# Key-value products of an item ahead of its second scores, with the copies, roundings and rests around the first layer pair and the gates put in another order

## The reference

```python
# 1: retention, B=2 batches, H=8 heads, S=768 steps, D=64
state = gamma * state + einsum('bhd,bhe->bhde', k[:, :, t], v[:, :, t])
y[:, :, t] = scale * einsum('bhd,bhde->bhe', q[:, :, t], state)
# 2: token mixing of rank 32 (U, V), then a two-layer MLP 512 -> 2048 -> 512
u = x + (x^T @ U @ V)^T
x2 = u + max(u @ w_ch1, 0) @ w_ch2
# 3: spatial gating
h = max(x2 @ w_in, 0); u3, v3 = h split in halves
v_s = w_spatial @ layernorm(v3) + b_spatial
out = (u3 * v_s) @ w_out
```

## Time and profile before

| | |
|---|---|
| median of 3 runs | 475.24 us (474.47 to 475.42) |
| the profiled execution | 473.94 us, its span 471.9 us |
| TensorE matmuls | busy 462.0 us, 98% of the span |
| VectorE | busy 339.2 us, 72% |
| ScalarE | busy 251.4 us, 53% |
| GpSimd | busy 48.2 us, 10% |
| the chain that ended last | 91% TensorE, 5% VectorE, 2% ScalarE, 2% transfers |

### The profile page before, as it was taken

One profiled execution on the slowest core, in us unless ns is written; L12 is line 12 of the kernel. 1 busy time (PEld: TensorE's weight loads), 2 busy tenths in 40 slices (PEclk: granted clock), 3 DMA queues, 4 the chain that ended last, 5 costly groups with the idle time before them and its releaser, 6 DMA issues.

```text
span 471.9 us, 8650 instructions
## 1 busy us (share of the span) xinstructions
PE 462.0 (98%) x3140; PEld 411.5 (87%) x3140; DVE 339.2 (72%) x755; ACT 251.4 (53%) x589; POOL 48.2 (10%) x52
## 2 busy tenths in 40 slices
PE   8899998999999999999999999999999999999997
PEld 5788897988999999988888999988888689999997
DVE  4788978887789987874855976774813997794430
ACT  1666755555667655833464655733432855454312
POOL 2178970000000000000100000000100001000000
PEclk9999999999999999999999999999999999999999
DMA  8989801344432343202220343202105002011003
GB/s 282 405 289 315 303 2 45 112 158 133 135 123 91 100 139 121 91 11 78 90 90 1 107 138 115 91 7 84 44 1 200 1 0 92 0 66 69 0 1 135
DMA packets 20361, 50.31 MB, mean 107 GB/s; under 512 B 1504, under 2 KB 3168, under 8 KB 19168
## 3 DMA queue, kind: packets, MB, share of 16 engines
q1 hardware_dynamic: 19904, 49.24, 30.4%
q10 hardware_dynamic: 416, 0.53, 0.3%
HBM read 46.61 MB, written 3.15 MB: 105 GB/s over the span
## 4 chain that ended last, share of the span: by engine, by line
PE 91%; DVE 5%; ACT 2%; DMA 2%; issue 1%; DVEq 0%; ACTq 0%
PE bank L1413 9%; PE bank L1411 9%; PE bank L1414 9%; PE bank L1394 8%; PE bank L1392 8%; PE bank L1395 8%; PE bank L1532 5%; PE bank L1261 3%; PE bank L1513 3%; PE bank L1516 3%; PE bank L1515 3%; PE bank L1451 2%; PE bank L1453 2%; PE bank L1452 2%; PE bank L1306 2%; PE bank L1300 2%
## 5 line engine op out<-in xcount | busy, mean ns | idle before, releaser
L1392 PE MATMUL bank<-bh,w1c 128*128 128x256 f32 x336 | 94.6, 282 | 1.9 <-DVE hl L985 1.9
L1395 PE MATMUL bank<-bh,w1c 128*128 128x256 f32 x336 | 94.7, 282 | 0.0
L1394 PE MATMUL bank<-bl,w1c 128*128 128x256 f32 x336 | 94.6, 282 | 0.0
L1413 PE MATMUL bank<-hl,w2h 128*128 128x512 f32 x192 | 75.9, 395 | 0.0
L1411 PE MATMUL bank<-hh,w2h 128*128 128x512 f32 x192 | 75.8, 395 | 0.0
L1414 PE MATMUL bank<-hh,w2l 128*128 128x512 f32 x192 | 74.7, 389 | 0.0
L1392 PEld LDWEIGHTS bank<-bh,w1c 128*128 128x128 f32 x336 | 63.5, 189 | 8.7 <-issue 2.1
L977 DVE TENSOR_TENSOR c<-bank,p 128x256 f32<-128x256 f32 x72 | 30.5, 424 | 52.6 <-PE bank L1395 31.4
L1394 PEld LDWEIGHTS bank<-bl,w1c 128*128 128x128 f32 x336 | 63.4, 189 | 5.5
L1395 PEld LDWEIGHTS bank<-bh,w1c 128*128 128x128 f32 x336 | 63.4, 189 | 0.0
L614 ACT ACTIVATE p<-bank 128x256 f32<-128x256 f32 x72 | 27.5, 381 | 48.2 <-PE bank L1395 47.1
(11 more groups left out here) (142 smaller groups left out, 933.2 us busy)
## 6 DMA issues: line engine op xcount, KB each, us to landing
w1raw<-w SPq DMA_DIRECT2D x24, 512.0 KB, 5.0
w2raw<-w SPq DMA_DIRECT2D x24, 512.0 KB, 4.1
att<-attn SPq DMA_DIRECT2D x7, 1152.0 KB, 7.8
att<-attn SPq DMA_DIRECT2D x10, 384.0 KB, 5.4
out_T<-stage SPq DMA_DIRECT2D x7, 384.0 KB, 2.4
wsp_raw<-w_sp SPq DMA_DIRECT2D x1, 2304.0 KB, 8.3
winraw<-w_in SPq DMA_DIRECT2D x4, 512.0 KB, 5.0
tab<-decay SPq DMA_DIRECT2D x7, 258.0 KB, 4.8
```

The source lines that it names most:

```text
L1392: mm(o, w1c[k][:, 0, q, s], bh[:, q, c, :], start=(opens and c == 0), stop=False, skip_group_check=True)
L1394: mm(o, w1c[k][:, 0, q, s], bl[:, q, c, :], start=False, stop=False, skip_group_check=True)
L1395: m = mm(o, w1c[k][:, 1, q, s], bh[:, q, c, :], start=False, stop=(c == 1), skip_group_check=True)
L1413: mm(ch_ps[c][:, :], w2h[h][:, s], hl[k][:, h, :], start=False, stop=False, skip_group_check=True)
```

## The change

Only orders and wait counts change; every engine does the same operations on the same tiles. (1) Items 2 to 7: kv(i) goes ahead of scores(i, 1) on TensorE, and states(i) ahead of mask_a(i, 1) on VectorE. (2) First pair: the third piece of the hidden tile (s=2, the one that sits in PSUM) is rounded and rested second, and product(1, 1) waits for two rests instead of three (HID_FIRST gives the new counts); rests of weights 4 to 6 of pair 1, p_rest(7) and u_add(7) go behind sum_c(1, 0) or later; up(7) moves from behind product(1, 0) to behind product(1, 4), and ch2(0, 0) from behind product(1, 1) to behind product(1, 2). (3) relu_in of the last stretch's tiles 0 and 1 goes ahead of round_wsp(0) and round_wsp(1). (4) For gates a = 0 and 2, sp_copy(a+1, 0) goes ahead of round_g(a, 3).

```diff
--- before.py
+++ after.py
@@ -283,6 +283,7 @@
             return kv_ps[:, c * P:(c + 1) * P] if c < NC - 2 else y_ps[1][:, GW:GW + P]
 
 
+        HID_FIRST = (1, 3, 2)
         WIN_AT = ((0, 4), (0, 5), (0, 6), (1, 3))
         PAIRS = NI // B
         NN = NT * NP
@@ -694,7 +695,9 @@
                     copy_pr(n, 0)
                     if n == 0:
                         xn_copy(NI - 1, 1)
-                    elif n > 1:
+                    elif n == 1:
+                        round_w1(n, range(4, NQ))
+                    else:
                         round_w2(n - 1, 1)
                     if n:
                         round_w1(n + 1, range(0, 2))
@@ -703,8 +706,9 @@
                     copy_pr(n, 1)
                     if n == 0:
                         copy_pr(n, 2)
+                    round_w1(n + 1, range(2, 4))
+                    if n == 0:
                         p_round(NI - 1)
-                    round_w1(n + 1, range(2, 4))
                     if final:
                         round_b(t + 1, range(1, 3))
                     if n:
@@ -721,12 +725,12 @@
                         round_b(t + 1, range(4, 5))
                     if t and j == 4:
                         round_x2(t - 1, range(2, 4))
+                    if n == 0:
+                        relu_hid(n, 2)
                     relu_hid(n, 1)
                     if n:
                         round_w2(n, 0)
-                    relu_hid(n, 2)
-                    if n == 0:
-                        round_w1(n + 1, range(4, 7))
+                        relu_hid(n, 2)
                     if final:
                         round_b(t + 1, range(5, 7))
                     if t and j >= 4:
@@ -808,9 +812,9 @@
             round_x2(NT - 1, range(1, CT))
             round_v(0, range(4, NQ))
             set_bias(0, 0)
+            relu_in(NT - 1, range(0, 2))
             round_wsp(0)
             round_wsp(1)
-            relu_in(NT - 1, range(0, 2))
             round_wsp(2)
             relu_in(NT - 1, range(2, 3))
             round_wsp(3)
@@ -824,7 +828,8 @@
             relu_in(NT - 1, range(6, 8))
 
             for a in range(NA):
-                sp_copy(a, 0)
+                if a % 2 == 0:
+                    sp_copy(a, 0)
                 if a:
                     set_bias(a, 1)
                 if a < NA - 1:
@@ -844,6 +849,8 @@
                 round_g(a, 2)
                 if a == 0:
                     round_wout(range(2, CT))
+                if a % 2 == 0:
+                    sp_copy(a + 1, 0)
                 round_g(a, 3)
                 if a == 1:
                     round_v(2, range(NQ))
@@ -978,7 +985,7 @@
 
             def rest_hid(n, s):
                 k = n % 2
-                dve.wait_ge(hid_hi, 3 * n + s + 1)
+                dve.wait_ge(hid_hi, 3 * n + s + 1 if n else HID_FIRST[s])
                 o, x, hi = ((hl[k][:, 1, HT:TW], c22[:, :], raw(hh[k])[:, 1, HT:TW]),
                             (hl[k][:, 0, :], c1[:, :], raw(hh[k])[:, 0, :]),
                             (hl[k][:, 1, 0:HT], pr_ps[k][:, 0:HT], raw(hh[k])[:, 1, 0:HT]))[s]
@@ -1043,9 +1050,12 @@
                                             ALU.subtract).then_inc(ust_lo, 1)
                 xn_rest(i - 1, 0)
                 xn_rest(i - 1, 1)
-                mask_a(i, 1)
+                if i == 1:
+                    mask_a(i, 1)
                 states(i, 0, NC - 2)
                 states(i, NC - 2, NC - 1)
+                if i > 1:
+                    mask_a(i, 1)
                 p_rest(i - 1)
                 if i == 1:
                     dve.wait_ge(vraw_loaded, 16)
@@ -1064,6 +1074,9 @@
                     if t and j == 1:
                         add_x2(t - 1, range(CT))
                     sum_c(n, 0)
+                    if n == 1:
+                        rest_w1(n, range(4, NQ))
+                        p_rest(NI - 1)
                     if t and j == 0:
                         rest_b(t, range(5, NQ))
                     if n == 0:
@@ -1075,7 +1088,7 @@
                     if n == 0:
                         sum_c(n, 1)
                         sum_c(n, 2)
-                        p_rest(NI - 1)
+                        rest_hid(n, 0)
                     weight_sums(n + 1, range(3, 4))
                     if final:
                         rest_b(t + 1, range(0, 1))
@@ -1088,17 +1101,17 @@
                         rest_w1(n + 1, range(4, 5))
                         sum_c(n, 2)
                         rest_w1(n + 1, range(5, 6))
-                    rest_hid(n, 0)
                     if n:
+                        rest_hid(n, 0)
                         rest_w1(n + 1, range(6, 7))
-                    else:
-                        rest_w1(n + 1, range(2, 4))
-                    rest_hid(n, 1)
-                    if n:
+                        rest_hid(n, 1)
                         rest_w2(n, 0)
                     rest_hid(n, 2)
                     if n == 0:
-                        rest_w1(n + 1, range(4, 7))
+                        rest_w1(n + 1, range(2, 3))
+                        rest_hid(n, 1)
+                        rest_w1(n + 1, range(3, 4))
+                    if n == 1:
                         u_add(NI - 1)
                     if final:
                         rest_b(t + 1, range(2, 5))
@@ -1352,9 +1365,12 @@
                 scores(i, 0)
                 turn(i - 1, 0)
                 turn(i - 1, 1)
-                scores(i, 1)
+                if i == 1:
+                    scores(i, 1)
                 kv(i, 0, NC - 2)
                 kv(i, NC - 2, NC - 1)
+                if i > 1:
+                    scores(i, 1)
                 down(i - 1)
                 outputs(i, 0)
                 outputs(i, 1)
@@ -1375,7 +1391,7 @@
                 if n and q == 0:
                     pe.wait_ge(c_sum, 3 * n)
                 if n and q == 1:
-                    pe.wait_ge(hid_lo, 3 * n)
+                    pe.wait_ge(hid_lo, 3 * n if n > 1 else 2)
                 if q == 2:
                     pe.wait_ge(pr_copied, 3 * n + 1)
                 if q == 3:
@@ -1399,7 +1415,7 @@
                 h, c = g // CT, g % CT
                 k, j = n % 2, n % NP
                 if c == 0:
-                    pe.wait_ge(hid_lo, 3 * n + 2 + h)
+                    pe.wait_ge(hid_lo, 3 * n + 2 + h if n else 3)
                     if n == 0:
                         pe.wait_ge(w2_first_lo, h + 1)
                     else:
@@ -1470,10 +1486,14 @@
                         continue
                     product(n, 0)
                     if n == 1:
-                        up(NI - 1)
-                    for q in range(1, 7):
+                        product(n, 1)
+                    for q in range(2 if n == 1 else 1, 7):
                         product(n, q)
-                        ch2(n - 1, q - 1)
+                        if n == 1 and q == 4:
+                            up(NI - 1)
+                        ch2(n - 1, q - (2 if n == 1 else 1))
+                    if n == 1:
+                        ch2(n - 1, 5)
                     ch2(n - 1, 6)
                     ch2(n - 1, 7)
                     if t and j == 4:
```

## The result

| | median | lowest to highest | executions |
|---|---|---|---|
| before | 475.33 us | 474.47 to 475.61 | 4 |
| after | 468.61 us | 468.33 to 469.25 | 4 |

The ratio is 0.9863, 95% interval [0.9846, 0.9881]: 6.7 us faster. The forecast was 471.4 us with a range of 470.2 to 472.9, so the change is faster, as forecast, but by more than the range allowed. The profiled execution took 468.76 us (span 466.7), against 473.94 (span 471.9) before: 5.2 us. That is less than the 6.7 between the medians, and both are more than the 3.85 of the sum.

What follows compares the result with a forecast made beforehand. TensorE's matmuls, filling 462.0 of 471.9 us, were taken as the bound. Terms 0.60 + 1.4 + 0.95 + 0.9 = 3.85 us off the profiled 473.94 gave 470.1; 1.30 added for the median made 471.4, range 470.2 to 472.9.

Steps and rivals of the forecast that it cites:

- 1 items: Items 3 and 7: kv ahead of the second scores covers TensorE's gaps of 0.41 and 0.19; 0.60 us, from 0 to 0.8.
- 2 first pair: Between pairs 0 and 1: product(1, 1) starts 1.91 us earlier, less 0.52 for moved up(7); 1.4 us, from 1.1 to 1.86.
- 3 input product: Last stretch's input product: TensorE's 0.92 us wait for a relu behind two roundings closes; 0.95 us, from 0.6 to 1.1.
- 4 gates: spatial(1): TensorE no longer waits for a copy queued behind round_g(0, 3); 0.9 us, from 0.5 to 0.96.
- The signs named ahead: Changed profile if right: hidden-tile wait 0.4 to 0.6 us, relu and copy waits gone, items' step 1.5 to 1.6, span 468.0.
- signs of being wrong: TensorE waiting on items 5-7 masks, pair 1 sum_c or weight rests, spatial rests, late VectorE sums, or over 0.3 in pairs 2-23.
- A: Items: shifted masks meet decay_q, making VectorE or GpSimd late again, so part 1 gives nothing; 472.0 us, chance 0.12.
- B: First pair: the gap moves to waits at product(1, 2) to (1, 6); 472.3 us, chance 0.10 with or without A.
- C: Input product and gates: VectorE's chain sets the pace, 1.85 us of gains mostly given back; 473.2 us, chance 0.06.
- D: Items: decay_q and masks collide in every item, costing 4.9 us; 476.9 us, slower, chance 0.03.
- E: More than forecast, as items 2 and 6 and restarts after gaps count too; 470.6 us, chance 0.66 together with the forecast.

Runs made afterwards that it cites:

- f3: Kernel before with 13 pairs of useless small matmuls filling the 1.86 us pause: ratio 1.0002, 474.04 us, none of 12 executions at the lower clock.
- g1: Kernel before with 8 instead of 13 pairs of useless small matmuls in the pause: ratio 0.9987, 473.55 us, none of 12 executions at the lower clock.
- e2: Kernel before with only the first pair's new order: ratio 0.9961, 472.00 us, none of 11 executions at the lower clock.
- f1: The changed kernel, unedited, repeated beside the kernel before on a second chip: ratio 0.9902, 469.16 us against 473.63 at like clock.
- g2: Kernel before with only the input product's relus moved ahead of the roundings: ratio 0.9983, 472.69 us at the higher clock.
- g3: Kernel before with only the spatial-weight copies moved ahead of round_g for gates 0 and 2: ratio 0.9989, 472.74 us at the higher clock.
- e3: Kernel before with both the relus and the spatial-weight copies moved, items and first pair untouched: ratio 0.9972, 471.75 us at the higher clock.
- e1: Kernel before with only the new order in items 2 to 7: ratio 0.9986, 473.06 us against 473.49 at like clock.

## Why the prediction was wrong

**The step that failed** is the one behind the sum: "The median of the runs shown, 475.24, is 1.30 above that execution, so the median should come to 471.4." It treats the distance between a profiled execution and the median as a constant that the change leaves alone. It was not: behind the change the median of 468.61 lies 0.15 below the profiled 468.76. In the forecast's own terms the miss of 2.8 us (471.4 against 468.61) is 1.45 from this step (1.30 and 0.15), 0.65 from terms sized too low, and about 0.7 because the profiled execution of before started late (22.04 against 21.35). The profiled execution of before (473.94, mean granted clock 0.999, forty nines on its page) had no fall of the clock; of the four runs of before, 475.24, 475.42 and 475.61 lie where on the other chips only executions with the fall lie (those without it end at 474.53), and 474.47 may be either. The clocks of these other runs are not recorded, so this reading is argued and not shown; that the pause makes the fall, and that either cure removes it, is shown by f3, g1, e2 and f1. On this reading the 1.30 was mostly the cost of a pause that the change closes, and should have been taken off. With the fall's cost counted (1.2 to 1.7 us by the groups), the same sum gives 475.24 - 3.85 - 1.2 to 1.7 = 469.7 to 470.2, at and under the range's lower end.

**The terms**, by the traces from scores(2, 0) on (449.86 to 445.35, 4.5 us) and by the repeats at like clock (4.47):

| term | forecast | trace | alone, like clock |
|---|---|---|---|
| 1 items | 0.60 | 0.90 | 0.43 |
| 2 first pair | 1.4 | 1.56 | 1.49 (and 1.66) |
| 3 input product | 0.95 | 1.08 | 1.06 |
| 4 gates | 0.9 | 0.96 | 1.01 |
| sum | 3.85 | 4.50 | 4.0 |

Each mechanism was right and each size a little low. In (1) items 3 and 7 give 0.40 and 0.18, as summed; items 2 and 6, left out of the sum with up to 0.2 in the range, give 0.11 each, and items 4 and 5 0.05 each, where outputs had waited shortly for the states. The 0.43 of part 1 alone is low beside the 0.89 of its own trace. In (2) the row "0.52" of the up-products is a duration; in the row of the changed kernel the next matmul starts 0.35 later, and this is what the moved work costs here. The gap came out as computed: 0.47 us. (3) was the whole difference of start times, 2.89 - 1.81, and the upper bound of 1.1; (4) its upper bound of 0.96. Together 0.65 us. In the repeat, the medians over all executions are 473.82 and 469.16, 4.66 us apart: only 5 of 18 executions of before had the fall there, so its median hardly holds it. The first comparison's 6.7 is then 4.5 of closed gaps, 1.2 to 1.7 for the fall if three of its four runs of before had it, and 0.5 to 1.0 that stays open: a start as in the profiled pair (0.69) or the chip would do, and nothing run here tells these apart. How many of four executions have the fall is luck, and so is that part of the miss.

**The signs named ahead.** The step from transposes to second scores is even, 1.53 to 1.54 us in items 2 to 7. The rest of the hidden tile is listed with 0.3 us, not 0.4 to 0.6 (from start to start it is 0.47), and the span is 466.7, not 468.0. None of the signs of being wrong came.

**The rivals.** A is out: the first mask of item 7 is done 0.3 us before TensorE wants it, about the 0.25 computed, and no wait on GpSimd is listed. B is out: product(1, 2) to (1, 6) follow without a gap, sum_c(1, 1) is done by 79.2. C is out: g2 and g3 alone and e3 together hold their gains. D is out: e1 is not slower, and decay_q got shorter, not longer (median 1011 ns against 1206, longest 1506 against 1723). E, more than forecast, was the case, at 470.6 still 2 us too high. What was missing is a rival that no row of the profile of before shows: an execution that loses clock behind a pause. That the profiled execution lay 0.5 us below the lowest of the three runs shown was the only sign.

## What to carry to other kernels

Treat a profiled execution's distance to the median as a term to be explained, not as a constant: look at each pause of the matmul engine of a microsecond or two ahead of dense work, and read the granted clock of several executions, not of one. When such a pause can't be closed, matmuls without use, placed in it, kept the clock here (0 of 24 executions fell, against 42%); they must end before the next real one, since 26 of them outlasted the pause and cost 0.4 us. Cost moved matmuls by start-to-start steps and gaps by the same, not by durations, and compare traces from a point behind the start-up.

## What the hardware did that I had not expected

One pause of 1.86 us of TensorE, in a kernel in which it is otherwise busy 98% of the time, was followed in 62 of 148 executions by a fall to half the clock (from 76.5 to 79.9 us in e1_items) while TensorE was at full work again. In the three profiled executions that had it, it set in 0.5 us (e3_relu_gates), 1.2 us (g3_gates) and 1.4 us (e1_items) after the restart. It costs 1.2 to 1.7 us by the groups' medians and 1.5 to 1.6 by the traces. A pause of 1.24 us in the same place had no such effect in 6 executions, which is too few to call it safe. On the page of the profile (here of e1_items), the fall is one digit (8 for 9) in the row of the granted clock of forty slices:

```profile
PEclk9999998999999999999999999999999999999999
```

The changed kernel and both filled ones have forty nines.
